# Fused chunk attention and two MLPs on one core: order and buffers of the first loads, place of the fifth group's transposes, steps of the first tile's attention visits

## The reference

```python
scores = scale * np.matmul(q_c, k_c.transpose(0, 1, 2, 4, 3))
attn = np.exp(scores - np.max(scores, axis=-1, keepdims=True))
attn = attn / (np.sum(attn, axis=-1, keepdims=True) + 1e-09)
x = merge_heads(np.matmul(attn, v_c))          # 4608 x 512
y = np.maximum(x @ w_in_a, 0.0) ** 2 @ w_out_a    # 512 -> 2048 -> 512
h = y @ w_in_b
g = np.where(h >= 1, h, np.where(h <= -1, 0.0, (h + 1) ** 2 / 4))
out = g @ w_out_b
```

## Time and profile before

| | |
|---|---|
| median of 3 runs | 1686.17 us (1685.52 to 1689.07) |
| the profiled execution | 1687.67 us, of which the span of the profile is 1685.87 (page: 1685.9) |
| mean granted TensorE clock | 0.997 |
| TensorE matmul busy | 1663.6 us |
| VectorE busy | 870.1 us |
| ScalarE busy | 621.8 us |
| GpSimd busy | 129.6 us |

### The profile page before, as it was taken

The page is one execution under the profiler, slowest core; times in us unless marked ns, Lnnn a source line. Parts: engine busy times, 40 slices in busy tenths (PEclk is TensorE's granted clock), DMA queues, the critical chain, the costliest instruction groups (busy, mean ns, idle before and its releaser), DMA issues.

```text
span 1685.9 us, 22430 instructions
## 1 busy us (share of the span) xinstructions
PE 1663.6 (99%) x8276; PEld 1374.4 (82%) x8276; DVE 870.1 (52%) x1626; ACT 621.8 (37%) x1425; POOL 129.6 (8%) x138
## 2 busy tenths in 40 slices
PE   6899999999999999999999999999999999999999
PEld 6788888888888888888888888888888888888887
DVE  4766676676667666665123444444444444343433
ACT  4564444443444344444453222222222222222222
POOL 2660000000000000000472000000000000000000
PEclk9999999999999999999999999999999999999999
DMA  7442121121212121121232010101010101000000
GB/s 145 119 119 63 26 57 38 26 68 27 65 38 58 25 63 39 26 57 32 101 99 77 1 51 0 51 1 50 0 50 0 50 0 50 0 30 21 14 12 25
DMA packets 126651, 74.62 MB, mean 44 GB/s; under 512 B 115552, under 2 KB 115552, under 8 KB 124256
## 3 DMA queue, kind: packets, MB, share of 16 engines
q1 hardware_dynamic: 119328, 56.11, 12.5%
q0 software_dynamic: 5120, 16.78, 3.4%
q10 hardware_dynamic: 2112, 0.52, 0.2%
HBM read 54.53 MB, written 18.87 MB: 44 GB/s over the span
## 4 chain that ended last, share of the span: by engine, by line
PE 97%; DVE 1%; ACT 1%; DMA 1%; SPq 0%; issue 0%; POOL 0%
PE h_ps L349 46%; PE acc L382 23%; PE acc L386 23%; PE heads_out_ps L448 2%; PE scores_ps L417 2%; PE h_ps L360 0%; SPq L183 0%; DMA qk_in<-in_q_dram 0%; DMA qk_in<-in_k_dram 0%; DVE q_t_and_k_t_by_head L687 0%; DVE v_and_probs_diag L756 0%; PE acc L448 0%; PE acc L401 0%; DVE hidden_split L784 0%; ACT probs L535 0%
## 5 line engine op out<-in xcount | busy, mean ns | idle before, releaser
L349 PE MATMUL h_ps<-x_t_split,w_in_split 128*128 128x512 f32 x3432 | 824.4, 389 | 0.4 <-issue 0.4
L349 PEld LDWEIGHTS h_ps<-x_t_split,w_in_split 128*128 128x128 f32 x3432 | 644.1, 188 | 134.6 <-issue 0.8
L382 PE MATMUL acc<-hidden_split,w_out_split 128*128 128x512 f32 x1728 | 419.5, 392 | 0.8 <-DVE hidden_split L784 0.8
L386 PE MATMUL acc<-w_out_split,hidden_split 128*128 128x512 f32 x1728 | 415.1, 389 | 0.9 <-DVE hidden_split L784 0.9
L382 PEld LDWEIGHTS acc<-hidden_split,w_out_split 128*128 128x128 f32 x1728 | 321.7, 188 | 72.5 <-issue 6.9
L386 PEld LDWEIGHTS acc<-w_out_split,hidden_split 128*128 128x128 f32 x1728 | 324.2, 188 | 68.5 <-ACT hidden_split L588 1.3
L784 DVE TENSOR_TENSOR hidden_split<-hidden_raw,hidden_split 128x512 fp32r<-128x512 f32 x288 | 199.6, 693 | 320.7 <-ACT hidden_split L588 320.6
L779 DVE SCALAR_TENSOR_TENSOR hidden_raw<-hidden_raw 128x512 f32<-128x512 f32 x144 | 99.6, 692 | 351.7 <-ACT hidden_raw L583 351.7
L588 ACT CAST hidden_split<-hidden_raw 128x512 fp32r<-128x512 f32 x288 | 178.8, 621 | 218.1 <-DVE hidden_raw L782 213.5
L578 ACT ACTIVATE hidden_raw<-h_ps 128x512 f32<-128x512 f32 x144 | 86.1, 598 | 425.5 <-PE h_ps L349 422.8
L583 ACT ACTIVATE hidden_raw<-h_ps 128x512 f32<-128x512 f32 x144 | 86.1, 598 | 367.6 <-PE h_ps L349 367.6
(11 more groups left out here) (67 smaller groups left out, 452.8 us busy)
## 6 DMA issues: line engine op xcount, KB each, us to landing
qk_in<-in_q_dram SPq DMA_DIRECT2D x72, 128.0 KB, 3.1
v_and_probs_diag<-in_v_dram SPq DMA_DIRECT2D x72, 128.0 KB, 3.0
mlp_out_t<-stage SPq DMA_DIRECT2D x9, 1024.0 KB, 4.3
v_and_probs_diag<-mlp_out_t SPq DMA_DIRECT2D x9, 1024.0 KB, 7.0
qk_in<-in_k_dram SPq DMA_DIRECT2D x68, 128.0 KB, 3.1
out_dram<-stage SPq DMA_DIRECT2D x8, 1024.0 KB, 5.1
stage<-in_moe_w_in_dram POOLq DMA_DIRECT2D x16, 256.0 KB, 3.2
stage<-in_moe_w_out_dram POOLq DMA_DIRECT2D x16, 256.0 KB, 3.4
```

The lines of the kernel that those rows point to most:

```text
L349: last = nc.tensor.matmul(h_ps[:, bank, :], w_in[:, kt, w, cols], x_t[:, par, x, kt, :], start=(kt == 0 and w == HI and x == HI), stop=(kt ...
L382: last = nc.tensor.matmul(acc[:, j, :], w_out[:, f, w, cols], hid[:, half, x, :], start=first, stop=end)
L386: last = nc.tensor.matmul(acc[:, j, :], hid[:, half, w, cols], w_out[:, f, x, :], start=first, stop=end)
```

## The change

The two first q and k loads of each of groups 0 and 1 are issued by SP and the other two by ScalarE, q first, and group 0's q has a semaphore of its own, so that its q can be transposed before its k is there. Group 2 is loaded into rows 1 and 3 of `stage`, a third buffer, without a wait; group 3 goes into slot 0 and group 4 into slot 1, each after a wait, and SP's order becomes qk 0, 1, 2, v 0, (wait for `turn(0)`) qk 3, v 1, v 2, (wait for `turn(1)`) qk 4, v 3, qk 5 (after `turn(4)`), v 4, v 5. GpSimd issues `load_in(0)` after `turn(1)`, ahead of `normalise(0)`, and `load_out(0)` after `turn(2)`, ahead of `normalise(2)`. `WARM` is 7. On TensorE `turn_probs(3)` follows `turn_probs(2)`, and group 4's transposes come after both first halves and `head_out(3)`. Group 4 uses `shift`, one exponential and `add_up` in tile 0 in place of `find_max` and `exponentials`. In tile 0 the visits come at steps 4, 8, 12 and 15; the other tiles keep theirs.

```diff
-WARM = 10
+WARM = 7
+STEPS_OF_FIRST_TILE = {1: (0, (0,)), 2: (0, (1,)), 3: (0, (2,)), 4: (0, (3,)), 5: (1, (0,)), 6: (1, (1,)), 7: (1, (2,)),
+                       8: (1, (3,)), 9: (2, (0,)), 10: (2, (1,)), 11: (2, (2,)), 12: (2, (3,)), 13: (3, (0, 1)),
+                       14: (3, (2,)), 15: (3, (3,))}
+def group_and_parts(t, f):
+    if isinstance(t, int) and t == 0:
+        return STEPS_OF_FIRST_TILE.get(f, (0, ()))
+    return f // QUARTER, (f % QUARTER,)
...
+        def qk_of(g):
+            if g == 2:
+                return stage[:, 1:4:2, :]
+            return qk_in[:, 0 if g in (0, 3) else 1, :, :]
...
 @block.sync
-                    if g >= 2:
-                        sp.wait_ge(k_turned, g - 1)
+                    sp.wait_ge(k_turned, 5 if g == EARLY else 4)
...
-            load_qk(0, 0)
-            load_qk(1, 1)
-            load_qk(2, 0)
+            for g in range(2):
+                for which, blocks in ((0, q_blocks), (1, k_blocks)):
+                    sp.dma_start(qk_of(g)[0:CHUNK, which, :].rearrange("t (h d) -> t h d", d=D),
+                                 blocks[0, 2 * g]).then_inc(first_q_loaded if (g, which) == (0, 0) else qk_loaded[g], DMA)
+            load_early_qk(2, staged_qk_loaded)
             load_v(0, 0)
-            load_qk(3, 1)
+            sp.wait_ge(k_turned, 1)
+            load_early_qk(3, qk_loaded[0])
             load_v(1, 1)
-            load_qk(4, 0)
             load_v(2, 0)
+            sp.wait_ge(k_turned, 2)
+            load_early_qk(4, qk_loaded[1])
             load_v(3, 1)
             load_qk(5, 1)
...
 @block.gpsimd
+            pool.wait_ge(k_turned, 2)
+            load_in(0, 0, stage)
             normalise(0, 0)
-            load_in(0, 0, stage)
+            load_in(1, 0, stage)
             normalise(1, 1)
-            load_in(1, 0, stage)
+            pool.wait_ge(k_turned, 3)
+            load_out(0, 0, stage)
             normalise(2, 0)
-            load_out(0, 0, stage)
...
 @block.tensor, tile
-                    if attends and f % QUARTER == QUARTER - 1:
-                        g = f // QUARTER
+                    g, parts = group_and_parts(t, f)
+                    if attends and QUARTER - 1 in parts:
                         head_out(GROUPS * (t + 1) + g, g % 2)
...
             turn_probs(2)
-            turn(GROUPS)
-            up_half(0, 0)
             turn_probs(3)
             head_out(2, 0)
+            up_half(0, 0)
+            head_out(3, 1)
             up_half(1, 0)
-            head_out(3, 1)
+            turn(GROUPS)
...
 @block.scalar
-                        exponentials(GROUPS, 0)
+                        exponentiate(GROUPS)
...
+            copy_turned(3)
             x_in_hi(2, 0, 2)
-            copy_turned(3)
...
 @block.vector, tile
-                    if attends and r == 0 and not begins:
+                    if attends and 0 in parts and not late:
                         normalise(n, g % 2)
...
                     if attends and begins:
-                        find_max(n, 0)
-                    if attends and first:
+                        shift(n)
+                        turn(t, 1, 1, TURNS[0], TURNS[1])
+                    if attends and 0 in parts and late:
+                        add_up(n, 0)
                         normalise(n, 0)
-                        turn_probs(n, 0)
...
-            x_in_lo(1, 0, 1)
+            for g in range(1, GROUPS):
+                x_in_lo(g, 0, g)
             copy_k(GROUPS, True)
-            x_in_lo(2, 0, 2)
-            x_in_lo(3, 0, 3)
```

More of the change, by code:

```diff
@@ L170, in _, with load_early_qk @@
         def _(sp):
+            def load_early_qk(g, loaded):
+                for j in range(2):
+                    c = 2 * g + j
+                    for which, blocks in ((0, q_blocks), (1, k_blocks)):
+                        sp.dma_start(
+                            qk_of(g)[j * CHUNK:(j + 1) * CHUNK, which, :].rearrange("t (h d) -> t h d", d=D),
+                            blocks[c // CPB, c % CPB]).then_inc(loaded, DMA)
             def load_qk(g, par):
                 if not past(g, EARLY + 2):
-                    if g >= 2:
-                        sp.wait_ge(k_turned, g - 1)
+                    sp.wait_ge(k_turned, 5 if g == EARLY else 4)
                 else:
@@ L180, in load_qk @@
                     for which, blocks in ((0, q_blocks), (1, k_blocks)):
-                        if which == 1 and not past(g, 2):
-                            continue
                         sp.dma_start(
@@ L392, in turn @@
             def turn(g):
-                pe.wait_ge(qk_loaded[g % 2], QK_DMAS * DMA * (g // 2 + 1))
                 if g > 0:
@@ L398, in turn @@
                 for which, turned in ((0, q_turned), (1, k_turned)):
+                    if g == 0 and which == 0:
+                        pe.wait_ge(first_q_loaded, 2 * DMA)
+                    elif g == 0:
+                        pe.wait_ge(qk_loaded[0], 2 * DMA)
+                    elif g == 2:
+                        pe.wait_ge(staged_qk_loaded, QK_DMAS * DMA)
+                    else:
+                        pe.wait_ge(qk_loaded[0 if g == 3 else 1], {1: 4, 3: 6, 4: 8}[g] * DMA)
                     for hp in range(HP):
                         cols = slice(hp * P, (hp + 1) * P)
-                        last = nc.tensor.transpose(acc[:, which, cols], qk_in[:, g % 2, which, cols], ident[:])
+                        last = nc.tensor.transpose(acc[:, which, cols], qk_of(g)[:, which, cols], ident[:])
                     last.then_inc(turned, 1)
@@ L624, in _ @@
             for g in range(2):
-                for j in range(2):
-                    c = 2 * g + j
-                    act.dma_start(qk_in[j * CHUNK:(j + 1) * CHUNK, g, 1, :].rearrange("t (h d) -> t h d", d=D),
-                                  k_blocks[c // CPB, c % CPB]).then_inc(qk_loaded[g], DMA)
+                for which, blocks in ((0, q_blocks), (1, k_blocks)):
+                    act.dma_start(qk_of(g)[CHUNK:2 * CHUNK, which, :].rearrange("t (h d) -> t h d", d=D),
+                                  blocks[0, 2 * g + 1]).then_inc(first_q_loaded if (g, which) == (0, 0) else qk_loaded[g], DMA)
             copy_q(0)
@@ L673, in x_in_lo, with turn @@
                                         x_t[:, half, HI, :, cols].bitcast(F32), ALU.subtract).then_inc(x_lo, 1)
-            def turn(n, par, begin, end):
+            def turn(t, k, par, begin, end):
+                n = GROUPS * (t + 1) + k
                 if begin == 0:
-                    dve.wait_ge(qk_loaded[par], QK_DMAS * DMA * (n // 2 + 1))
+                    dve.wait_ge(qk_loaded[par], 2 * QK_DMAS * DMA * t + DMA * (QK_DMAS * (2 + k // 2) + (-2 if par == 0 else 4)))
                     dve.wait_ge(scored, n)
@@ L741, in normalise @@
                 dve.wait_ge(inverted, n + 1)
-                if not past(n, GROUPS):
+                if not past(n, EARLY):
                     dve.wait_ge(normed, n)
@@ L764, in tile @@
                     a = raw[:, half, :]
-                    g, r = divmod(f, QUARTER)
+                    g, parts = group_and_parts(t, f)
                     n = GROUPS * (t + 1) + g
                     begins = not past(t, 1) and f == 0
-                    first = not past(t, 1) and f == 1
-                    if attends and r == 0 and not begins:
+                    late = not past(t, 1) and g == 0
+                    if attends and 0 in parts and not late:
                         normalise(n, g % 2)
-                    if attends and r in (1, 2) and not first:
-                        turn_probs(n, r - 1)
-                    if attends and r == 3 and not ends(t, g + 1):
+                    for r in (1, 2):
+                        if attends and r in parts:
+                            turn_probs(n, r - 1)
+                    if attends and 3 in parts and not ends(t, g + 1):
                         find_max(n + 1, (g + 1) % 2)
@@ L797, in tile @@
                         nc.vector.tensor_copy(stage[:, 3, :], acc[:, 3, :]).then_inc(acc_dve, 1)
-                    if attends and r == 3:
+                    if attends and 3 in parts:
                         x_in_lo(n, 1 - par, g)
                         if not ends(t, g + 2):
-                            turn(n + 2, g % 2, TURNS[0], TURNS[1])
-                    if attends and r < 3 and not ends(t, g + 1):
-                        turn(n + 1, (g + 1) % 2, 0 if begins else TURNS[r + 1], TURNS[r + 2])
+                            turn(t, g + 2, g % 2, TURNS[0], TURNS[1])
+                    for r in range(3):
+                        if attends and r in parts and not ends(t, g + 1):
+                            turn(t, g + 1, (g + 1) % 2, TURNS[r + 1], TURNS[r + 2])
                     if not attends and X_STEP <= f < X_STEP + KT:
```

13 lines of the change are left out of this document (6 added, 7 removed).

## The result

Over all its runs the changed kernel took 1678.18 us (median of 6, 1677.49 to 1680.56), the kernel before, over as many, 1689.19 (1685.52 to 1691.47). The ratio is 0.9942, 95% interval [0.9928, 0.9955]. Three more sets put the kernel before at 1688.23, 1688.88 and 1687.92, and the changed one, run again, at 1678.24 (ratio 0.9935 [0.9917, 0.9953]). So the change is worth about 10 us, 0.6%, clear of the 0.2% bound (the two medians are 11.0 us apart, the ratio gives 9.8). I had forecast 11.8 us and 1674.4: 3.8 too low, of which 2 to 3 is the base (the three runs shown gave 1686.17, later sets 1688 to 1689) and 1 to 2 the gain.

What follows compares the result with a forecast made beforehand. TensorE was taken as the bound, busy 1663.6 of 1685.9 us with 22.3 us idle at the start. Gains of 8.5 + 3.3 = 11.8 us from 1687.67 gave 1675.9, less 1.5 to the median: 1674.4 us, range 1671.3 to 1679.0.

Steps and rivals of the forecast that it cites:

- Part 1, the loads: Start: group 3's last load lands at 16.7 us, so `turn(3)` and the chain behind it start 1.4 us earlier (0 to 1.9).
- rival 1: Start: loads stay the limit and group 3 lands at 18.0 as before; loses 1.4 us, giving 1675.8; chance 0.12.
- Part 2, `turn(4)`: Start: `turn(4)` after `head_out(3)` frees `turn_probs(3)` 3.5 us earlier; with the loads, `down(0, 0)` comes 8.5 us earlier, at 39.0.
- The hole: TensorE between `turn_probs(2)` and `turn_probs(3)`: 2.9 us with nothing to do; 1.5 us charged for the clock (nothing to 3.5).
- Part 3, tile 0: Tile 0, from `down(0, 0)`: the visit after `up(0, 4)` leaves 1.5 us stall, saving 3.3 us (2.0 to 4.4).
- GpSimd's holds: VectorE in tile 0: the inverse step and a subtraction can be held by GpSimd; 1.1 us taken, up to 1.1 + 1.3 more.
- Group 5's loads: Tile 0: they land at 41.0 to 41.8, within VectorE's 1.3 us slack, costing nothing; at 7.1 us latency, 2.3 us.
- my 12.1: VectorE's queue in tile 0, first subtraction to end of third: 12.1 us, against 11.72 when TensorE asks for it.
- Rival 2: Group 5's or V 3's loads are late, or GpSimd holds VectorE longer: 2.3 + 1.3 + 1.0 us less, 1679.0; chance 0.13.
- Rival 3: Start: the shorter warm-up leaves the clock at half through groups 0 and 1, about 0.9 us each on three steps: 1677.1; chance 0.07.
- 4: The new hole drops TensorE's clock and it stays down: slower, 1690 us or above; chance 0.03.
- rival 5: Tile 0: VectorE's queue becomes the pace from step 1 and hands every gain back, about 1685 us; chance 0.05.

Runs made afterwards that it cites:

- experiment 9: The changed kernel run again, unedited, against the kernel before in a later set: 1678.24 us, ratio 0.9935.
- 12: Changed kernel with the edits of 10 and 11 together, and `load_v(3, 1)` issued ahead of group 4's loads: 1672.72 us, ratio 0.9906 to the kernel before.
- experiment 2: Changed kernel with ten identity matmuls on TensorE filling the hole between `turn_probs(2)` and `turn_probs(3)`: 1679.83 us, ratio 0.9932 to the kernel before.
- Experiment 3: Changed kernel with TensorE's old order in the start, `turn(4)` and `up_half(0, 0)` ahead of `turn_probs(3)`: 1688.06 us, ratio 0.9991 to the kernel before.
- experiment 1: Changed kernel with VectorE making group 5's first three q/k blocks in step 1 of tile 0, not step 0: 1678.42 us, ratio 0.9932 to the kernel before.
- experiment 5: Changed kernel with the slots of groups 3 and 4 exchanged, so group 5's loads wait for `turn(3)`: 1678.92 us, ratio 0.9936 to the kernel before.
- 6: Changed kernel with ten warm-up matmuls instead of seven: 1678.56 us, ratio 0.9936 to the kernel before.
- 10: Changed kernel with ten warm-up matmuls and ten more in the hole before `turn_probs(3)`: 1679.07 us, ratio 0.9943 to the kernel before.
- Experiment 4: Changed kernel with tile 0's visits at steps 3, 7, 11, 15 as before, group 4's parts packed into steps 1 to 3: 1685.22 us, ratio 0.9981.
- 7: Changed kernel with VectorE's subtraction ahead of group 4's probability blocks in steps 2 and 3 of tile 0: 1680.5 us, ratio 0.995 to the kernel before.
- 8: Changed kernel with GpSimd's subtractions for weight slices 2 to 5 made for an eighth of their columns: 1677.66 us, ratio 0.993 to the kernel before.
- 11: Changed kernel, tile 0 visits at steps 5, 8, 12, 15, VectorE's subtraction first, group 5's blocks in steps 2 to 4: 1675.95 us, ratio 0.9921.

## Why the prediction was right and wrong

**Direction and place were right:** faster, clear of noise, with the gain in the first 40 us. That the total came within 2 us is partly luck: a term of 3.3 us came to nothing, and the medians differ by 2 to 3 us more than the profiles, 7.9 us, which is all that was forecast from.

**Part 1, the loads.** I took 1.4 us (0 to 1.9). Measured 0.66, with group 3's last load down at about 17.3, not 16.7, as some of SP's issues took 1.0 to 1.3 us where I had 0.64: the last of group 3 was out at 12.09, not at 10.4. In experiment 9 the term was 1.26, in 12 1.9. In 2 and 3, which lost time at half clock before, `turn(3)` came at 19.02 and 18.93, later than in the kernel before (18.07), and below my lower bound. So the bounds were right where the clock held. 0.66 lies between rival 1's no gain and my value, 1.26 near mine.

**Part 2, `turn(4)`.** 8.5 us forecast at `down(0, 0)`, 8.1 measured, 8.0 in experiment 9. `turn_probs(3)` started at 26.32 (25.6). The hole came as said, 2.92 us (2.9), and the clock fell behind it, to 0.50 from 27 to 29 us: `turn_probs(3)` took 1.97 us where 1.15 is usual, and `head_out(2)` 1.85 for 1.05, 1.6 us in all. I had charged 1.5. From `up_half(1, 0)` to `down(0, 0)` it was 6.79 (6.8). Experiment 3 shows that this part carries the gain, given the new load order: without it the whole median gain goes. `load_v(3)`, which I had late "by up to 1 us", made `head_out(3)` wait in seven of the profiles of changed kernels (0.67 to 1.91 us), mostly those where the clock held before it; not in the first.

**Part 3, tile 0, is the step that failed:** "Stall 1.5 (0.4 to 2.8), saving 4.83 - 1.5 = 3.3 us". Up to `down(0, 2)` the stall was 53.37 - 39.38 - 10.88 = 3.1 us, twice that, and the half clock behind it took 1.6 more. With what hand-overs add the loss was 4.9, so the saving was nothing. Three terms:
- *GpSimd's holds*, of which I took 1.1 out of "between nothing and 1.1 + 1.3 more". I had the inverse step and one subtraction; the second and the fourth subtraction and the inverse step were held, by 0.6, 0.7 and 1.1 us, of which 1.7 us fell before the end of the third. Making GpSimd's operations small took 1.9 us off.
- *Group 5's loads*, priced at "nothing; were it the 7.1 of the earlier trace rows, 2.3 us". They landed at about 42.98, not 41.0 to 41.8, and VectorE was ready at 40.7: 2.30 us of wait, 1.2 beyond the slack until 43.15, when ScalarE's copy was there. With the 1.7 of holds this makes up the 2.6 us by which the queue overran my 12.1, within 0.3. It cost the 0.67 us before `down(0, 1)` (gone in experiment 1). What more it cost is open: experiment 1 put the blocks elsewhere in the same queue, and in experiment 5 ScalarE was late.
- *The clock in tile 0*, which I had not charged at all. In the kernel before it was full (1.00) from 46 to 70 us, though TensorE waited 1.80 and 1.82 us there; here, after 0.67 + 1.90 us of waits, it fell, at a cost of 1.6 us. It fell in all seven profiles with seven warm-up matmuls and a wait of 1.88 us or more in tile 0, and in neither of the two with ten (6 and 10), at the same waits. Whether the warm-up has to do with it or chance, two profiles do not tell.

Experiment 4 corrects how I had read the change: I set the later visits against the old stalls, 4.83 us. Against the stalls that the new start makes they are worth 7 us, half clock included, and all of it goes to pay for what the new start adds to VectorE's queue.

**The base.** The median of the three runs shown was about 2 us below that of later sets.

**Rivals.** Rival 2 (loads late, VectorE held longer, 1679.0) is what happened in kind and nearly in size. Rival 3 was set too low: with seven warm-up matmuls the profiled executions of experiments 2, 3, 7, 8 and 11 ran `score(0)` or the transposes behind it at half clock, five of ten; with ten, none of three (6, 10, 12), which is too few to be sure that the warm-up decides it. Experiment 6's median is that of the changed kernel; there group 0's scores start 0.9 us later, which may cost what the clock gives. Rivals 1 and 4 did not come: group 3 was earlier where the clock held, and the clock came back (1.00 from 30 us). Of rival 5 the mechanism came, but it took back only what tile 0 was to give; the visits at 8, 12 and 15 were without a wait.

**The spread.** Executions of one kernel differ by 5 us and more, and their mean granted clock goes with it. In the last set the kernel before took 1685.74 us at 0.998, 1686.83 to 1687.92 at 0.997, 1688.50 to 1690.84 at 0.996, 1692.32 at 0.995 and 1694.38 at 0.994: about 2 us for each thousandth. The changed kernel's executions are mostly at 0.998 to 1.000. With two thousandths between the middle executions (0.997 and 0.999), an estimated 4 us at most of its gain in the medians is time no longer spent at half clock; the profiled pair, 0.997 and 0.998, shows half of that. The mean does not see everything: experiment 2's profile ran the first groups at times of the half clock under a row of 1.00.

Left open: what decides in which executions the clock falls, at the start, behind the hole and in tile 0, and what group 5's late loads alone cost.

## What to carry to other kernels

When a bound engine's path is shortened, price the queue of the engine that feeds it from the first instruction to the new deadline, with the holds by its neighbour as a measured row and not as a tail; here one step more until the visit (5.44 us) was worth more than any reordering in that queue. A load order and an order of use are one change: the loads without the order of use made the kernel no faster than before. And where a wait is removed, look for the engine that was just as late behind it, before moving loads for it.
